# Attention ahead of an MoE: x stays in SBUF, another order on ScalarE and TensorE, and GpSimd takes part

## The reference

```
a      = softmax over m of phi                     # phi: 8 x 8 x 576 x 32
k_m, v_m = einsum('bhsm,bhsd->bhmd', a, k), ... v  # 32 memory slots per head
attn   = softmax over m of (q @ k_m^T) / 8         # sums + 1e-9 in both
x      = attn @ v_m, heads side by side            # 4608 tokens x 512
h      = x @ w_in;  g = h * sigmoid(1.702 h);  x2 = g @ w_out      # 512 -> 2048 -> 512
per token: the expert (of 8) with the largest x2 @ w_gate,
out    = p(expert) * sigmoid(output gate) * (relu(x2 @ w1[e]) @ w2[e])
```

## Time and profile before

| | |
|---|---|
| Median of 3 runs | 1362.95 us |
| Profiled execution | 1360.2 us, span in the profile 1358.1 us |
| Granted clock of TensorE, mean | 0.998 |
| Busy over the span | PE 1321.8 us, DVE 660.8, ACT 388.8, POOL 527.6 |
| Chain that ended last | 93% PE |
| Attention, first scores to last | 15.54 to 115.92 us |
| DMA in 60 to 80 us | 406 GB/s |

### The profile page before, as it was taken

One profiled execution on the slowest core, in us unless ns is written; L12 is line 12 of the kernel. 1 busy time (PEld: TensorE's weight loads), 2 busy tenths in 40 slices (PEclk: granted clock), 3 DMA queues, 4 the chain that ended last, 5 costly groups with the idle time before them and its releaser, 6 DMA issues.

```text
span 1358.1 us, 25712 instructions
## 1 busy us (share of the span) xinstructions
PE 1321.8 (97%) x7778; PEld 1075.4 (79%) x7779; DVE 660.8 (49%) x1349; ACT 388.8 (29%) x721; POOL 527.6 (39%) x622
## 2 busy tenths in 40 slices
PE   6888999999999999999999999999999999999997
PEld 4566788888888888888888888887788888888886
DVE  5997243453433433434334344347655555555553
ACT  3554222232222222322223222223322222222221
POOL 2005774453344433433434435511433342433331
PEclk9999999999999999999999999999999999999999
DMA  8996447656565465454654646547873779649882
GB/s 322 391 409 251 139 153 206 201 193 184 189 193 182 160 192 188 169 186 155 185 193 159 184 175 192 176 148 258 238 226 96 219 227 266 169 125 250 259 238 62
DMA packets 155641, 275.28 MB, mean 203 GB/s; under 512 B 17107, under 2 KB 54244, under 8 KB 153540
## 3 DMA queue, kind: packets, MB, share of 16 engines
q1 hardware_dynamic: 98804, 205.35, 44.0%
q10 hardware_dynamic: 43600, 37.37, 11.2%
q0 software_dynamic: 13184, 31.88, 7.5%
HBM read 146.03 MB, written 100.45 MB: 181 GB/s over the span
## 4 chain that ended last, share of the span: by engine, by line
PE 93%; DMA 2%; POOL 1%; ACT 1%; issue 1%; DVE 0%; ACTq 0%; SPq 0%; POOLq 0%; DVEq 0%
PE ps L674 28%; PE ps L707 28%; PE ps L748 16%; PE ps L777 15%; PE ps L633 2%; PE ps L620 1%; PE ps L648 1%; PE ps L717 1%; DMA x2x<-xT_scratch 1%; DMA raw<-in_moe_w_out 1%; PE ps L605 1%; DMA kvm<-in_kv 1%; DMA xT_scratch<-xo 1%; POOL W L1509 0%; POOL xs L1538 0%
## 5 line engine op out<-in xcount | busy, mean ns | idle before, releaser
L674 PE MATMUL ps<-xs,W 128*128 (+1 forms) x1728 | 417.8, 391 | 3.1 <-POOL W L1519 1.6
L707 PE MATMUL ps<-W,gs 128*128 128x512 f32 x1728 | 415.0, 389 | 0.1
L674 PEld LDWEIGHTS ps<-xs,W 128*128 128x128 f32 x1728 | 322.8, 188 | 73.0 <-issue 4.4
L707 PEld LDWEIGHTS ps<-W,gs 128*128 128x128 f32 x1728 | 324.2, 188 | 67.9 <-DVE gs L1205 0.5
L1203 DVE TENSOR_TENSOR gate<-ps,gate 128x512 f32<-128x512 f32 x144 | 99.6, 691 | 358.8 <-ACT gate L931 358.4
L931 ACT ACTIVATE gate<-ps 128x512 f32<-128x512 f32 x144 | 86.1, 598 | 466.3 <-PE ps L674 465.8
L748 PE MATMUL ps<-W,cx 128*128 (+1 forms) x936 | 218.5, 389 | 0.8 <-issue 0.8
L777 PE MATMUL ps<-W,chT 128*128 (+1 forms) x936 | 218.3, 389 | 0.9 <-DVE chT L1340 0.9
L1546 POOL CAST whi<-raw 128x512 fp32r<-128x512 f32 x128 | 85.4, 667 | 319.0 <-DMA raw<-in_moe_w 318.9
L777 PEld LDWEIGHTS ps<-W,chT 128*128 128x128 f32 x936 | 175.5, 188 | 38.1 <-issue 1.7
L748 PEld LDWEIGHTS ps<-W,cx 128*128 128x128 f32 x936 | 175.5, 188 | 37.6 <-issue 1.4
(11 more groups left out here) (158 smaller groups left out, 810.4 us busy)
## 6 DMA issues: line engine op xcount, KB each, us to landing
W<-expert_scratch SPq DMA_DIRECT2D x24, 2048.0 KB, 11.0
raw<-in_moe_w SPq DMA_DIRECT2D x128, 256.0 KB, 2.8
expert_scratch<-whi SPq DMA_DIRECT2D x128, 256.0 KB, 2.6
expert_scratch<-raw SPq DMA_DIRECT2D x128, 256.0 KB, 2.9
cq<-ch ACTq DMA_DIRECT2D x156, 128.0 KB, 3.8
kvm<-in_kv SPq DMA_DIRECT2D x16, 1152.0 KB, 7.1
crec<-record_scratch POOLq DMA_DIRECT2D x160, 64.0 KB, 3.7
qT<-in_q SPq DMA_DIRECT2D x16, 576.0 KB, 6.3
```

The lines of the kernel that those rows point to most:

```text
L674: mm = pe.matmul(ps[:, f % 2, :], W[:, col:col + P], xs[:, bass.ds(x0 + (x_lo * K1 + c) * T, T)], start=(c == 0 and w_lo + x_lo == 0), sto ...
L707: mm = pe.matmul(ps[:, 2 + s, :], gs[:, f % 2, g_lo, s * P:(s + 1) * P], W[:, col:col + DM], start=(f == 0 and g_lo + w_lo == 0), stop=(f ...
```

## The change

In attention:

- k, v and phi are laid out by blocks of 128 tokens (four, and one of 64), so that the transposes of `aT` are 4 of 128 x 128 and 2 of 64 x 64 (18 of 64 x 64 before), and the k/v products 16 with 128 rows and 4 with 64 (36 with 64 rows before).
- k and v are scaled together (`kv_scale`), and POOL makes the v blocks (`v_blocks`) and the multiplication by the inverse sums (`normalize`), all but the last. DVE treats the phi sum and the score sums in one addition and one inverse (`inverses`). The scores have two buffers `sc`.
- x goes to a tile `keep` in SBUF, in the place of weights that are split later. All batches but the last two are stored to `xT_scratch` by two DMAs in group 15, the seventh by two after it, the last by one.
- The first x tile is split from `keep`: the high part by ACT in group 15 (`first_x_hi`), the low part three times by POOL and once by DVE.
- ACT, PE and DVE have another order of steps in a group.

The diff, cut to its core:

```diff
             def load_qkv(g, b, u):
                 wait(sp, s_kv, g - 1)
-                sp.dma_start(kvm[u][:].rearrange("p w h n -> p (w h n)"), kv[bass.ds(g * P, P), :]).then_inc(s_kvl[u], 16)
+                sp.dma_start(kvm[u][:], kv[bass.ds(g * P, P), :]).then_inc(s_kvl[u], 16)
...
-                if not isinstance(g, int) or g >= 4:
-                    store_group(g, b, u)
...
+            def a_transposes(g):
+                wait(pe, s_aT, g + 1)
+                for c in range(CA):
+                    pe.transpose(ps[:, 0, c * P:(c + 1) * P], aT[:, c * P:(c + 1) * P], ident[:])
+                for hh in range(2):
...
             def group(g, b, r):
+                wait(pe, s_kvl[u], 16 * (b + 1))
...
+                mm.then_inc(s_kv, 1)
+                if not last:
+                    a_transposes(g + 1)
                 wait(pe, s_kmT, g)
+                hold(pe, s_kk, g + 1)
+                for i in range(2):
+                    tr = pe.matmul(ps[i * D:(i + 1) * D, 1, 3 * P:4 * P], kvs[:, 0:D], ident[:],
...
                 if has_out:
                     out_half(g - 2, (r + 2) % 4, 0)
...
                 mm.then_inc(s_sc, 1)
+                if has_out:
+                    out_half(g - 2, (r + 2) % 4, 1)
...
+            mm1(0, 0)
             for i in range(2):
                 out_half(NG - 2, (NG - 2) % 4, i, (4, 2)[i])
-            mm1(0, 0)
...
+            def kv_scale(g, u):
+                wait(act, s_rin, g + 1)
+                wait(act, s_kv, g + 1)
                 wait(act, s_ktr, g)
+                wait(act, s_vbd, g)
+                act.activation(kvs[:], ps[:, 4, 3 * P:4 * P], ACT.Copy, scale=scs[:, u, 2, SB:SB + 1]).then_inc(s_kk, 1)
...
+            def store_kept(b, n, stored):
+                act.wait_ge(s_xo, 4 * (b + n))
+                for u in range(2):
+                    act.dma_start(xT_dram[2 * u * P:(2 * u + 2) * P, b * S:(b + n) * S].rearrange("(a p) n -> p a n", a=2),
+                                  keep_v[:, :, kept_at(b, u):kept_at(b + n, u)]).then_inc(stored, 16)
...
+            def inverses(g, u, scores, phi):
+                lo, hi = (0 if scores else SB), (SB + 1 if phi else SB)
+                if scores:
+                    wait(dve, s_ex, g - 1)
+                    dve.tensor_reduce(scs[:, u, 1, 0:SB], by_m(u), AX.X, ALU.add).then_inc(s_sm, 1)
...
             def group(g, b, r):
+                if not last:
+                    phi_in(g + 1, b + u, 1 - u)
+                inverses(g, u, two, True)
+                if not isinstance(g, int) or g:
+                    less_max(g - 1, 1 - u)
+                if two:
+                    attn_out(g - 2, u)
...
+            def normalize(g, u):
+                pool.wait_ge(s_rin, g + 3)
+                by_m = sc[u][:].rearrange("p (n m) -> p n m", m=M)
+                pool.tensor_tensor(by_m, by_m, scs[:, u, 2:3, 0:SB].rearrange("p o n -> p n o").broadcast_to([P, SB, M]),
+                                   ALU.mult).then_inc(s_nrm, 1)
...
+            for g in range(NG):
+                if g >= 2:
+                    normalize(g - 2, g % 2)
+                if g == NG - 1:
+                    for c in range(2):
+                        first_x_lo(c)
+                v_blocks(g, g % 4)
+                for c, at in enumerate((2, 3, NG - 4, NG - 3)):
+                    if g == at:
+                        split_w_in(c, c, 0)
+            first_x_lo(2)
+            normalize(NG - 2, 0)
+            pool.wait_ge(s_x3, 1)
+            pool.wait_ge(b_xlo, K1 - 1)
+            pool.sem_inc(b_xlo, 1)
```

More of the change, by code:

```diff
@@ L35 @@
 NG = B * H // HG
-CA = 9
-PA = S // CA
+CA = S // P
+PA = S - CA * P
 QA = S // M
@@ L116, in build @@
         sb("to_512", [P, 96 - RING * (NE + 4)])
+        with ExitStack() as a:
+            keep = sbt(a, "keep", [P, 2 * SLOT])
         W = sb("W", [P, 2 * SLOT], F32R)
@@ L612, in group @@
                 has_out = not isinstance(g, int) or g >= 2
-                wait(pe, s_aT, g + 1)
-                wait(pe, s_kmT, g)
-                hold(pe, s_vbd, g)
-                for c in range(CA):
-                    for hh in range(2):
-                        rows = slice(hh * PA, (hh + 1) * PA)
-                        tr = pe.matmul(ps[rows, c // 8, (c % 8) * 2 * M:(c % 8 + 1) * 2 * M], aT[rows, c * PA:(c + 1) * PA],
-                                       ident[rows, rows], start=True, stop=True, tile_position=(hh * PA, hh * PA))
@@ L622, in group @@
-                tr.then_inc(s_atr, 1)
+                last = isinstance(g, int) and g == NG - 1
+                wait(pe, s_kvl[u], 16 * (b + 1))
+                if not isinstance(g, int) or g >= 3:
+                    wait(pe, s_xo, 2 * g - 5)
+                hold(pe, s_am, g + 1)
+                out_of = lambda h: ps[h * M:(h + 1) * M, 4, 3 * P:4 * P].rearrange("p (w d) -> p w d", w=2)
+                for c in range(CA):
+                    for h in range(HG):
+                        pe.matmul(out_of(h), am[:, c * P + h * M:c * P + (h + 1) * M], kv_main[u][:, :, h, c, :],
+                                  start=(c == 0), stop=False, tile_position=(0, h * M))
@@ new lines, in group @@
+                for h in range(HG):
+                    hh, h2 = h // 2, h % 2
+                    rows = slice(hh * PA, (hh + 1) * PA)
+                    mm = pe.matmul(out_of(h), am[rows, CA * P + h2 * M:CA * P + (h2 + 1) * M], kv_left[u][rows, :, h2, :],
+                                   start=False, stop=True, tile_position=(hh * PA, h * M))
+                mm.then_inc(s_kv, 1)
+                if not last:
+                    a_transposes(g + 1)
+                wait(pe, s_kmT, g)
@@ L1154, in x_lo, with attn_out @@
+            def attn_out(g, u):
+                wait(dve, s_nrm, g + 1)
+                wait(dve, s_o, 2 * g)
+                dve.transpose(pT[:], sc[u][:]).then_inc(s_pT, 1)
             def x_lo(t, c):
```

291 lines of the change are left out of this document (141 added, 150 removed).

## The result

The changed kernel takes 1373.06 us (median of 5 runs, 1370.98 to 1375.89), the kernel before 1360.7 beside it (5 runs, 1359.34 to 1366.06). The ratio is 1.0086, 95% interval 1.0061 to 1.0112; it is worked out over all runs and so isn't exactly that of the two medians. The forecast was 1353 with a range to 1366: wrong in sign and outside of the range. The profiled execution has a span of 1371.4 us (before: 1358.1).

The account below looks back on a forecast made before the run. The prediction took a circle of latencies through four engines' queues to bound attention. Last scores 8.9 us earlier, less 0.9 for the handover, gave 8.0 us off 1360.2: 1352.2, forecast as 1353, range 1344 to 1366.

Parts of the forecast that it names:

- The circle: Attention: the loop of latencies through four engines' queues that sets a group's period falls from 6.52 to 5.3 us.
- DVE and POOL: Attention: DVE's work a group falls from 6.24 to 5.05 us; POOL's `normalize`, 1.46 us, hides and costs DVE 0.
- Rival C: Attention: DVE's subtraction waits for POOL's `normalize` over SBUF, at most 0.9 us a group; period 6.1, total 1359; chance 0.18.
- phi lands 4.2 us after the scores ended: Attention: phi's load, issued behind q's, holds DVE, so the period is 5.65 us instead of 5.3.
- +2 for chunks and `normalize`: Attention: weight chunks hinder phi's load three times and POOL's `normalize` up to four times, adding 2 us.
- rival D: Attention: the PE array stays at the lower clock and bounds at 7.4 us a group; total 1375; chance 0.05.
- step (a): Handover: through POOL's last `normalize` and eight chunks, `mm1(0, 4)` could start at 23.5 us, with 4 us of room.
- Rival W: Handover: weight chunks land behind the stores, `mm1(0, 4)` comes about 41 us after the last scores; total 1365; chance 0.13.
- Path (b): Handover: `g_step(0, 3)` waits for all stores, 27.1 us +0.4 to land, putting `mm2(0, 3)` 30.5 us after the last scores.

Follow-up runs that it names:

- `phi_filler`: The changed kernel with phi's load issued ahead of q's and four unread matmuls a group on PE: 1366.7 us, ratio 1.0025.
- `phi_first`: The changed kernel with phi's load issued ahead of q's in SP's order: 1366.5 us, ratio 1.0029.
- `split_later`: The changed kernel with POOL's splits of the first four weight chunks one group later, their loads unmoved: 1374.3 us, ratio 1.0081.
- `filler`: The changed kernel with four unread matmuls more a group on PE, where it waits for the scaled k: 1374.7 us, ratio 1.0079.
- `small_rows`: The changed kernel with the two stores of six batches each split into twelve DMAs of one batch: 1375.9 us, ratio 1.0102.
- `spread`: The changed kernel with the stores of the first six batches moved from group 15 back into the groups on SP: 1376.5 us, ratio 1.0107.
- `spread_ready`: The changed kernel with phi's load ahead of q's, four unread matmuls a group, four chunk splits one group later, stores in the groups: 1356.7 us, ratio 0.9953.

## Why the prediction was wrong

**The circle, right.** 5.53 us where phi is in time (5.3 forecast), and 5.4 with phi first; the 5.7 of the runs with unread matmuls is PE's own work. The exponential, the scaling and the transposed k follow each other as worked out.

**DVE and POOL, right.** The subtraction takes 0.76 us, `normalize` 1.16 (1.46 forecast). Rival C didn't come in the changed kernel: the two miss each other, and no subtraction took over 0.89 us. Where DVE and POOL do meet they cost what C said. In `phi_filler` a subtraction that started beside `normalize` took 1.23 us, and the split of a weight chunk, which I hadn't priced for this, made one of 1.65 in `phi_first`.

```profile
41.53 1.16 POOL L1567 TENSOR_TENSOR sc<-sc,scs 128x576 f32<-128x576 f32 x1
...
42.08 1.23 DVE L1166 TENSOR_TENSOR sc<-sc,scs 128x576 f32<-128x576 f32 x1
```

In each case, and in the earlier trace rows, the subtraction ends about 0.6 us after the POOL operation does. The Trainium skill (SBUF — State Buffer, Who interferes with whom) says that the port pair which the two engines share is an exclusive lock; these rows agree with it to within 0.15 us of the 0.76 that a subtraction takes alone.

**The step "phi lands 4.2 us after the scores ended": wrong size, right mechanism.** The scores end at 65.80 and DVE starts on phi at 71.51, 5.7 us later. Everything else of the term held: 5.2 us from the transposes to the end of the next scores (66.12 to 71.33), 1.95 from phi's maximum to the transposes (71.51 to 73.46). With 5.7 in its place the formula gives (5.2 + 5.7 + 1.95)/2 = 6.4 us instead of 5.65, some 10 us over 13 groups, most of the 11 that are missing. I had priced the landing by bytes of q and phi alone, at the full rate, with a latency from the best landing of the earlier trace rows, behind attention. Here the 1.18 MB of k and v are issued 1.5 us behind phi and 4.2 us ahead of q (61.84), and a landing takes 5.0 us in the median. That the k/v load shares the engines with phi is the likely reason, but wasn't tried by itself. The trace of before had a warning, in its list of DMA issues: phi's own loads took 7.3 us to land in the median, where I took 2.4 from the chunks.

```profile
phT<-in_phi SPq DMA_DIRECT2D x16, 288.0 KB, 7.3
```

**The step "+2 for chunks and `normalize`": of the wrong kind.** I priced a chunk by its 0.65 us of transfer. What `phi_filler` shows is a 4.3 us wait at the head of POOL's order, which now has `normalize` behind it, and 1.8 us of it on PE. While phi was late this cost next to nothing on top (`split_later`).

**The lower clock, rival D: there, in another form.** It came in stretches after a pause of PE, not for the whole of attention, and each stretch makes a pause a little longer: `filler` gains 1.5 us net of its own price, so the full cost in attention isn't known. In the handover it costs 1.6 us, in `mm1(0, 4)`, which no rival had. My condition for D (PE's work a group at the lower level over 6.63 us) was not what decided.

**The handover, step (a) "has 4 us of room for chunks that land later": wrong.** Rival W came, with a chance of 0.13. Two chunks were 8 and 10 us late and the rest in turn. W's own size was too large: it put `mm1(0, 4)` 41 us after the last scores, and it came at 34.6. (Its sum has slips as well: 41 is 14 us more than the 27.0 of before and not 13, and 9.44 MB at 406 GB/s are 23.3 us and not 23.7.) Path (b), on which I had built, held by itself: ACT starts `g_step(0, 3)` 26.8 us after the last scores (27.5 forecast), released by the stores.

```profile
144.76 0.60 ACT L978 ACTIVATE gate<-ps 128x512 f32<-128x512 f32 x1 [10.30 <-DMA xT_scratch<-xo]
```

The weights were later still, so that `mm2(0, 3)` started 8.5 us behind the forecast. I had dismissed W because stores of 0.59 MB had not stopped loads before; those were rows of 2.3 KB, and in `small_rows`, with rows of 2.3 KB, less than half of the delay was left (5.9 and 5.6 us to land, 2.5 to 2.9 with no burst in `spread`).

**What I had not asked: what the DMA engines do in the whole stretch.** Busy time of the kernel before in two stretches:

```profile
60.00:110.00 50.00, 43.90 (x1021) 30.54 (x1019) 46.39 (x101) 29.55 (x63) 2.27 (x2) 1.00 1.02 408
110.00:143.00 33.00, 28.65 (x250) 20.93 (x234) 19.27 (x30) 12.14 (x21) 24.97 (x24) 1.00 0.59 210
```

They ran at a share of 1.02, then of 0.59. Of the period of 6.52 us, 2.65 MB at 406 GB/s already made 6.5. The profile of before thus had two bounds on one line, the circle and the bytes. The change lifts the bound of the bytes by moving twelve stores of 0.59 MB, 7.1 MB, to the end; at 406 GB/s they need 17 us there, in a handover in which 0.41 x 33 = 13.5 us of DMA time were free. By this sum the two halves are one account, and `spread_ready` shows what a group gains when the bytes stay where they were: 6.45 instead of 6.63 us. The DMA share stands in the earlier trace rows, and I read it for one stage only.

## What to carry to other kernels

When a wait is taken out of a circle, look at what lands just in time for the old period, and price it by the landing times of its own loads in the same stage, not by the best of another. Stores that are moved off a busy stage are not gone: add up bytes over both stages, and look which small loads will stand beside or behind them, since an in-order engine that waits for one such load delays all that follow. An engine that gets a share of the critical path must have no wait for something else ahead of it in its order. And an edit that is made to measure something, like work put into a pause, has its own price: look whether the engine that got it has become the bound.
